# One core: a first head that prepares itself differently, and a last head whose weighted sum goes by halves

## What is computed

```python
# q, k, v: (2, 8, 768, 64), proj: (64, 6)
q_bits = (q @ proj > 0); k_bits = (k @ proj > 0)
mask = bucket(q_bits)[..., :, None] == bucket(k_bits)[..., None, :]
scores = where(mask, q @ k.T / 8, -1e9)
attn = softmax(scores); x = attn @ v            # -> (1536, 512)
logits = x @ w_gate                             # (1536, 8)
# by falling logit: a token goes to its expert while that has < 192 tokens
y[tok] = relu(x[tok] @ w1[e]) @ w2[e]           # w1: (8, 512, 1024), w2: (8, 1024, 512)
h = y @ w_in; out = (h * sigmoid(h)) @ w_out    # w_in: (512, 2048)
```

## Time and profile before

| what | value |
|---|---|
| three executions, median | 775.11 us (773.96 to 776.61) |
| the profiled execution | 777.72 us, span 775.9 us |
| mean granted TensorE clock | 0.990 |
| PE busy | 744.7 us (96%) |
| DVE busy | 481.1 us (62%) |
| ACT busy | 268.1 us (35%) |
| POOL busy | 156.4 us (20%) |

### The profile page before, as it was taken

How to read it: one execution, slowest core, us unless ns; L and a number is a source line. 1 busy time by engine, 2 the same in 40 slices (tenths; PEclk the granted TensorE clock), 3 DMA queues, 4 the chain that set the end, 5 groups by cost and what they waited for, 6 DMA issues and landing times.

```text
span 775.9 us, 19348 instructions
## 1 busy us (share of the span) xinstructions
PE 744.7 (96%) x7778; PEld 629.4 (81%) x7785; DVE 481.1 (62%) x1097; ACT 268.1 (35%) x551; POOL 156.4 (20%) x193
## 2 busy tenths in 40 slices
PE   8799999999998899999999999999999999999996
PEld 4577777777777569999999999978887888878885
DVE  4788888888889888797797740653233323242321
ACT  4768767767765012222222212221013101211111
POOL 5443545545643011010010000000002000010001
PEclk9899999999999899999999999999999999999999
DMA  7265565565533063463463477500001000010001
GB/s 151 46 121 119 123 139 118 122 139 126 114 106 86 22 236 112 137 219 136 137 206 149 136 247 277 183 0 1 1 1 54 0 0 0 0 54 0 0 0 54
DMA packets 58194, 75.07 MB, mean 97 GB/s; under 512 B 28736, under 2 KB 43072, under 8 KB 57120
## 3 DMA queue, kind: packets, MB, share of 16 engines
q1 hardware_dynamic: 54592, 67.12, 30.3%
q0 software_dynamic: 2208, 7.21, 2.9%
q10 hardware_dynamic: 1344, 0.04, 0.1%
HBM read 64.92 MB, written 6.29 MB: 92 GB/s over the span
## 4 chain that ended last, share of the span: by engine, by line
PE 86%; issue 4%; DVE 3%; DMA 2%; ACT 2%; POOL 1%; DVEq 0%; SPq 0%; ACTq 0%; POOLq 0%
PE quad_ps L1527 17%; PE quad_ps L1416 10%; PE quad_ps L1428 10%; PE quad_ps L1249 9%; PE score_ps L1510 8%; PE quad_ps L1510 8%; PE score_ps L1234 5%; PE score_ps L1235 4%; PE work_ps L1358 3%; PE work_ps L1220 2%; PE quad_ps L1258 2%; DMA area<-x_rows,ids_now 1%; DMA experts_w<-in_k 1%; PE pv_ps L1202 1%; DVE area L1030 1%
## 5 line engine op out<-in xcount | busy, mean ns | idle before, releaser
L1527 PE MATMUL quad_ps<-y_s,w_in_s 128*128 128x512 f32 x576 | 137.8, 390 | 2.7 <-DVE y_s L1152 2.0
L1527 PEld LDWEIGHTS quad_ps<-y_s,w_in_s 128*128 128x128 f32 x576 | 107.9, 188 | 26.2 <-DVE y_s L1152 2.8
L1170 DVE TENSOR_TENSOR gate<-quad_ps,sig 128x512 f32<-128x512 f32 x48 | 33.2, 692 | 145.9 <-ACT sig L656 145.9
L870 DVE TENSOR_SCALAR_CACHE_REDUCE att_area<-score_ps 128x768 f32<-128x768 f32 x96 | 91.9, 957 | 39.1 <-PE score_ps L1235 37.4
L524 ACT ACTIVATE att_area<-att_area 128x768 f32<-128x768 f32 x96 | 90.1, 939 | 46.0 <-DVE att_area L870 44.8
L656 ACT ACTIVATE sig<-quad_ps 128x512 f32<-128x512 f32 x48 | 28.7, 598 | 210.5 <-PE quad_ps L1527 210.5
L1416 PE MATMUL quad_ps<-area,experts_w 128*128 128x192 f32 x512 | 96.1, 334 | 1.5 <-ACT area L616 1.2
L1428 PE MATMUL quad_ps<-area,experts_w 128*128 128x192 f32 x512 | 87.2, 328 | 0.0
L1416 PEld LDWEIGHTS quad_ps<-area,experts_w 128*128 128x128 f32 x512 | 81.8, 190 | 2.1 <-ACT area L616 2.1
L1428 PEld LDWEIGHTS quad_ps<-area,experts_w 128*128 128x128 f32 x512 | 82.9, 190 | 0.0
L1234 PE MATMUL score_ps<-k_parts,q_parts 128*128 128x512 f32 x192 | 72.9, 380 | 10.3 <-DVE att_area L870 10.0
(11 more groups left out here) (204 smaller groups left out, 1104.6 us busy)
## 6 DMA issues: line engine op xcount, KB each, us to landing
experts_w<-in_moe_w SPq DMA_DIRECT2D x16, 2048.0 KB, 9.5
att_area<-in_v SPq DMA_DIRECT2D x64, 192.0 KB, 3.8
experts_w<-in_moe_w_in SPq DMA_DIRECT2D x8, 512.0 KB, 5.4
w_out_raw<-in_moe_w_out SPq DMA_DIRECT2D x4, 1024.0 KB, 8.3
experts_w<-in_k SPq DMA_DIRECT2D x16, 192.0 KB, 3.3
experts_w<-in_q SPq DMA_DIRECT2D x16, 192.0 KB, 3.6
k_bits<-k_parts SPq DMA_DIRECT2D x16, 192.0 KB, 4.6
x_rows<-att_area SPq DMA_DIRECT2D x8, 384.0 KB, 3.1
```

The lines of the kernel that those rows point to most:

```text
L870: nc.vector.tensor_scalar(probs[c % 3], score_ps[0][:, 0:S], 0.5 * BIG, None, ALU.min, ALU.min, accum_out=neg_max[:, c:c + 1]).then_inc(s_ ...
L1170: nc.vector.tensor_tensor(gate[:, :], layer_ps[f % 2][:, 0:GT], sig[:, :], ALU.mult).then_inc(s_mul, 1)
L1527: done = nc.tensor.matmul(layer_ps[f % 2][:, 0:GT], w_in_s[:, a, w_cols], y_s[:, c, b, :], start=(c == 0 and a + b == 0), stop=(c == DC - ...
```

## The change

Front: the high part of q of head 0 is written by ScalarE instead of GpSimd; the two transfers of the gate weights are started by SP, behind those of v; TensorE gets unread products in the slots of the first pair (`FIRST_UNREAD`, per head and slot). End of attention: the weighted sum of head 14 is shared out as 8, 8, 0, 8 blocks over slots 0 to 3 of the last head instead of 4, 4, 0, 12, 4; ScalarE copies it a slot earlier, and both copies of the best row come after that; the weighted sum of head 15 is made for tiles 0 to 2 and then for tiles 3 to 5 (96 columns a product instead of 192), the first half as soon as three tiles are transposed; its copy and `x_rows` go by halves too, and the copy stands ahead of ScalarE's six drains of head 14 (L588). GpSimd makes the last two splits of `w_in` one after the other, ahead of the logits of head 13. First ranking: unread products after rows 5 to 10 are 4, 4, 4, 3, 2, 0 instead of 4 each.

```diff
--- before.py
+++ after.py
@@ -412,6 +412,8 @@
             cross(0, k_drained(0))
             load_v(0, 0)
             load_v(1, 1)
+            for r0 in (0, D):
+                sp.dma_start(to_x[r0:r0 + D, :, D:DE], w_gate.rearrange("(h d) e -> d h e", d=D)).then_inc(s_wg, 16)
             cross(1, k_drained(1))
 
             def pair(g, write):
@@ -525,20 +527,21 @@
                                      bias=neg_max[:, c:c + 1],
                                      accum_out=row_sum[:, c:c + 1]).then_inc(s_exp, 1)
 
-            def turned(h):
+            def turned(h, ts=slice(0, T)):
 
                 act.wait_ge(s_pv, h + 1)
-                nc.scalar.activation(weighted_t.rearrange("p (t a j) -> p a t j", t=T, j=Q), sums_ps, ACT.Copy).then_inc(s_turned, 1)
+                dst = weighted_t.rearrange("p (t a j) -> p a t j", t=T, j=Q)
+                nc.scalar.activation(dst[:, :, ts, :], sums_ps[:, :, ts, :], ACT.Copy).then_inc(s_turned, 1)
 
             for i in range(4):
                 drain_work(PREP_KINDS[i], i % 2, i, 0)
+            act.wait_ge(s_work_free, 6)
+            nc.scalar.activation(q_bits[0][0:D, :], q_parts[0][0:D, :].bitcast(f32), ACT.Copy).then_inc(s_bit_step, 1)
             for t in range(2):
                 exp_tile(t, t)
                 for half in range(2):
                     drain_work("q" if t else "k", half, PREP + 2 * t + half, 1)
             act.wait_ge(s_halves, 5)
-            for r0 in (0, D):
-                act.dma_start(to_x[r0:r0 + D, :, D:DE], w_gate.rearrange("(h d) e -> d h e", d=D)).then_inc(s_wg, 16)
 
             def first_batch_row_out(c):
 
@@ -554,7 +557,7 @@
                     for t in range(T):
                         c = p * T + t
                         n = 2 * T * g + c
-                        if t == T - 1 and not (first and p == 0):
+                        if t == (T - 2 if last and p == 1 else T - 1) and not (first and p == 0):
                             if not first:
                                 act.wait_ge(s_x_full, 2 * g + p - 1)
                             turned(2 * g + p - 1)
@@ -565,8 +568,9 @@
                             w = w + 1
                         if len(ev[t]) < 2:
                             next_exp(n, c, last)
-                        if last and p == 1 and t >= T - 2:
-                            first_batch_row_out(t - (T - 2))
+                        if last and p == 1 and t == T - 2:
+                            first_batch_row_out(0)
+                            first_batch_row_out(1)
 
             def next_exp(n, c, last):
 
@@ -581,13 +585,14 @@
             none = assigned[:, 0, 0:1].unsqueeze(1).broadcast_to([P, NT, 2 * P - CAP])
             nc.scalar.activation(one_hot[:, :, CAP:2 * P], none, ACT.Copy).then_inc(s_cleared, 1)
             act.wait_ge(s_x_full, HEADS - 1)
+            for half in range(2):
+                turned(HEADS - 1, slice(half * (T // 2), (half + 1) * (T // 2)))
             act.wait_ge(s_xw, 16 * PAIRS)
             act.wait_ge(s_head_logits, HEADS - 1)
             for t in range(T):
                 col = t * DE
                 x_half = nc.scalar.activation(x_nat[:, t, 0:D], work_banks[0][:, col:col + D], ACT.Copy, scale=row_inv[:, t:t + 1])
             x_half.then_inc(s_x_free, 1)
-            turned(HEADS - 1)
 
             def second_batch_row_out():
 
@@ -733,8 +738,7 @@
 
             def finish_first_bits():
 
-                keep_high_of_q(0, 6)
-                pool.wait_ge(s_bit_step, 1)
+                hold(s_work_free, 6)
                 nc.gpsimd.tensor_scalar(k_bits[0][D:P, :], k_bits[0][D:P, :].bitcast(f32), -BIG, k_shift[D:P, :],
                                         ALU.mult, ALU.add).then_inc(s_bit_step, 1)
                 pool.wait_ge(s_bit_step, 2)
@@ -784,11 +788,10 @@
                     if not last:
                         split_rows(h + 2, p, g + 1)
                     if last and p == 1:
-                        split_beside(PAIRS - 2, h)
+                        for i in (PAIRS - 2, PAIRS - 1):
+                            split_beside(i, h)
                     if not first:
                         add_logits(h - 2)
-                    if last and p == 1:
-                        split_beside(PAIRS - 1, h)
                     if beside is not None and p == 0:
                         split_beside(beside, h)
 
@@ -1210,15 +1213,16 @@
                                             start=False, stop=True)
                 last.then_inc(s_work_full, 1)
 
-            def x_rows(h, bank, free=None):
+            def x_rows(h, bank, free=None, ts=range(T)):
 
                 rhs = to_x[:, h % H, :] if isinstance(h, int) else to_x[:, bass.ds(h % H, 1), :].rearrange("p a e -> p (a e)")
                 if free is not None:
                     pe.wait_ge(s_work_free, free)
-                pe.wait_ge(s_turned, h + 1)
-                for t in range(T):
+                pe.wait_ge(s_turned, h + 1 + (ts[0] > 0))
+                for t in ts:
                     last = nc.tensor.matmul(bank[:, t * DE:(t + 1) * DE], weighted_t[:, t * P:(t + 1) * P], rhs, start=True, stop=True)
-                last.then_inc(s_x_full, 1)
+                if ts[-1] == T - 1:
+                    last.then_inc(s_x_full, 1)
 
             def scores(c, h, n, crossed):
 
@@ -1236,20 +1240,20 @@
                                             start=False, stop=True)
                 done.then_inc(s_scores, 1)
 
-            def weighted(h, p, b0, n, loads):
+            def weighted(h, p, b0, n, loads, t0=0, t1=T):
 
                 if n and b0 == 0:
-                    pe.wait_ge(s_pt, T * h + T)
+                    pe.wait_ge(s_pt, T * h + t1)
                     pe.wait_ge(s_v[p], 64 * loads + 64)
                     pe.wait_ge(s_turned, h)
                 for b in range(b0, b0 + n):
                     for a in range(P // Q):
                         rows = slice(Q * a, Q * (a + 1))
                         side = slice(D * (b % 2), D * (b % 2 + 1))
-                        done = nc.tensor.matmul(quad_ps[side, 512 * a:512 * a + QT],
+                        done = nc.tensor.matmul(quad_ps[side, 512 * a + Q * t0:512 * a + Q * t1],
                                                 v_quarters[p][rows, b % 4, D * (b // 4):D * (b // 4 + 1)],
-                                                probs_t[p][rows, :, Q * b:Q * (b + 1)], start=(b < 2), stop=(b >= KB - 2))
-                if n and b0 + n == KB:
+                                                probs_t[p][rows, t0:t1, Q * b:Q * (b + 1)], start=(b < 2), stop=(b >= KB - 2))
+                if n and b0 + n == KB and t1 == T:
                     done.then_inc(s_pv, 1)
 
             def keep_busy(n, bank, cols=512):
@@ -1286,7 +1290,9 @@
                     if j in (3, T - 1):
                         done.then_inc(s_row_ps, 1)
 
+            FIRST_UNREAD = [[1, 1, 4, 4, 2, 2], [0, 0, 3, 0, 0, 0]]
             SHARE = [4, 4, 0, 12, 4, 0]
+            LAST_SHARE = [8, 8, 0, 8, 0, 0]
 
             def pair(g, first, last):
                 u = prep_base(g)
@@ -1304,19 +1310,27 @@
                             fill_work(kind, half, u - 1, h + ahead, (p + ahead) % 2, work_banks[half],
                                       x_free=h if kind == "k" and half == 0 and not first else None)
                             u = u + 1
+                        if first:
+                            if p == 1 and t == 2:
+                                pe.wait_ge(s_work_free, u - 1)
+                            keep_busy(FIRST_UNREAD[p][t], idle_bank if p == 0 else work_banks[0])
                         if t == 2 and not first:
                             x_rows(h - 2, work_banks[0], u - 1)
                         if last and p == 1 and t == T - 2:
                             row_of_first_batch(u)
                         if len(ev[t]) < 2:
-                            weighted_part(h, p, t, first, g)
+                            weighted_part(h, p, t, first, g, LAST_SHARE if last and p == 1 else SHARE)
+                        if last and p == 1 and t == T - 1:
+                            pe.wait_ge(s_row, 2)
+                            x_rows(HEADS - 2, work_banks[0])
+                            weighted(HEADS - 1, 1, 0, KB, PAIRS - 1, 0, T // 2)
                         if last and (p == 0 and t >= T - 2 or p == 1 and t < 2):
                             keep_busy(2, work_banks[1])
 
-            def weighted_part(h, p, t, first, g):
+            def weighted_part(h, p, t, first, g, share=SHARE):
 
                 if not (first and p == 0):
-                    weighted(h - 1, 1 - p, sum(SHARE[0:t]), SHARE[t], g if p else g - 1)
+                    weighted(h - 1, 1 - p, sum(share[0:t]), share[t], g if p else g - 1)
 
             pair(0, True, False)
             pe.wait_ge(s_wg, 32)
@@ -1324,10 +1338,9 @@
             with pe.Fori(1, PAIRS - 1, 1) as g:
                 pair(g, False, False)
```

(9 more changed lines are left out.)

## The result

The changed kernel takes 780.91 us (median of 5 runs, 779.9 to 782.94) against 775.11 (773.96 to 776.8, 5 runs) for the kernel before on the same chip: ratio 1.0071 [1.0054, 1.0088], 5.8 us slower. The profiled execution of after took 780.21 us, that of before 777.72, so the profiles hold only 2.5 us of difference; before's lies 2.6 above its median.

What follows compares the result with a forecast made beforehand. TensorE was seen busy nearly everywhere, with two 6.8 us stretches at 1.2 GHz. Front 2.2, copy and x_rows 0.3 and ranking 1.0 (half, for the median) make 3.5 us off 775.11: 771.6 us, range 770.0 to 774.6.

Steps and rivals of the forecast that it cites:

- Step 1: Front, high part of the first q on ScalarE: first scores start earlier, gain 0.25 us.
- Step 2: Front, gate weights issued from SP: ScalarE's drain of the k bits no longer waits for issues, gain 0.25 us.
- Step 3: Front, unread products in the first pair: they cost 0.2 us and gain 1.9 by removing the slow-clock stretch.
- rival (b): The low clock only moves, to the placing after the ranking: 773.5 us, or 775 if both places fall; chance 0.12.
- Step 4: Last head, shares 8, 8, 0, 8: scores slip 1.2 us, later slots give it back; net 0, bounds -0.3 and +0.7.
- Rival (d): The last head's slots hold back s_row by their 1.2 us: 772.8 us; chance 0.10.
- Step 5: GpSimd's last w_in splits together: last subtraction some 2 us earlier, not on the path; 0, up to 0.5 if logits late.
- Step 6: End of attention, head 15's weighted sum by halves: 4.1 us, as before; bounds 3.9 and 8.3.
- Rival (c): Weighted sum: a tile round keeps its length with halved columns, 8.3 us, kernel 775.8, or 777.1 at 25 ns; chance 0.10.
- rounds of over 0.12 us: Sign of a wrong forecast in head 15's weighted sum, where a round of eight was predicted at 0.085 us.
- Step 7: After head 15's sum, copy and x_rows by halves: gain 0.33 us, bounds 0 and 0.5.
- Step 8: First ranking, fewer unread products: `load` follows VectorE directly, gain 1.9 us, 0 without a slow clock, 1.0 for the median.

Runs made afterwards that it cites:

- e11_handed: `e1_front` without the unread products in the first pair, so only high part of q on ScalarE and gate weights on SP; 774.54 us, 0.9978 of before.
- e7_no_unread: `e2_whole` without the unread products in the first pair; 774.51 us, 0.9991 of before, twelve runs from 771.7 to 778.92.
- e1_front: The changed kernel with only its front part, end of attention and ranking as before; 774.45 us, 0.9987 of before.
- e6_twice: The changed kernel with head 15's weighted sum made twice over at full width (192 columns), no halves in it; 779.94 us, 1.0058 of before.
- e2_whole: The changed kernel with head 15's weighted sum in one go of 192 columns instead of halves; 773.04 us, 0.997 of before.
- e9_lean: `e2_whole` without unread products in the last head's first two slots; 772.33 us, 0.9948 of before, and again 771.94 us, 0.9945.
- e8_old_rank: `e2_whole` with the ranking's unread products as before, 4 after each of rows 5 to 10; 772.8 us, 0.996 of before.
- e4_halves: The kernel before with only head 15's weighted sum by halves of 96 columns; 778.73 us, 1.0041 of before.
- e5_filled: The changed kernel with 16 unread 512-column products spread through head 15's halves, one behind every 24 pairs; 782.9 us, 1.0098 of before.

## Why the prediction was wrong, step by step

- *Step 1* held. Scores start 2.96 us after the k bits' first drain instead of 3.23: 0.27 for a predicted 0.25.
- *Step 2* held: L520 follows its product without an issue. Its gain shows only without unread products, where the fourth and fifth minimum lie 2.36 us apart (`e11_handed`) instead of 2.55. In after it is 2.55 again: the unread products take the 0.19 back, as the 0.2 of step 3 allowed.
- *Step 3* held in the profile, 1.93 us for the whole front (predicted 2.2), of which the three tiles give 1.84 (1.9). It was mis-sized for the median: 1.1 us timed alone. The low clock of the one profiled execution isn't in all of them, and `e7_no_unread` kept its clock without the products, so it isn't shown that these are what keeps it. In `e1_front` a stretch fell on head 15's sum (the 5.85 us above). That is like rival (b), but neither at its place nor for its reason, since that kernel has the old products in the ranking.
- *Step 4* held: the slots slip by 1.30 (predicted 1.2) and give back 1.50. Rival (d) is out.
- *Step 5*: nothing of it is on the path, as said. GpSimd's last subtraction ends 4.8 us earlier (241.03), not 2, and VectorE's L883 takes 0.13 us at 242.09 instead of 2.09.
- *Step 6* is the step that failed: "4.1, as before", measured 9.20, above its own upper bound of 8.3. Its reasoning on the round was nearly right. Of the 45 rounds of eight inside the three runs 23 take 0.083 us, for a predicted 0.085; the others take 0.09 to 0.14, and the mean is 0.10. That makes 0.9 of the 5.05 us; the gaps make the rest (0.32 + 1.99 + 1.88 from start to start).
  What it left out is that the number of instructions doubles while the time for them doesn't, so that their supply becomes the bound. Rival (c) named the nearest time (775.8 to 777.1, with a chance of 0.10), still 3.8 us or more short, and by another mechanism, a fixed length of the round. That mechanism is refuted by the 0.083 us against 0.163 at full width (`e6_twice`). The sign I had set as wrong, "rounds of over 0.12 us", didn't occur in the mean. The 25 ns rule of the Trainium skill ("TensorE: Matmul & The Clock Gate", section "Wait — 56ns, not 53.3ns?") made it 9.6 us, close to the 9.20; the trace doesn't agree with it on these tiles, where pairs come 12.4 ns apart. The nearness is luck: the 9.20 comes from the supply's 27 ns a pair.
- *Step 7* held: sum's end to logits takes 2.31 us in `e2_whole` instead of 2.57, a gain of 0.26 (predicted 0.33). In after it is hidden by x_rows at 1.2 GHz: 2.84 us instead of 1.57.
- *Step 8* held in its mechanism: `load` follows right behind VectorE's last addition, L866. Its size is less sure. In `e2_whole` L1058 comes 13.97 us after the logits, 1.92 less (predicted 1.9), but that execution had no low clock there, and by the prediction itself the gain would then be 0. With one, at lengths like that of the earlier trace rows, this stretch of `e9_lean` takes 14.42 us from logits to `load`, 1.5 less than before:
```profile
255.80:263.00 7.20, 6.89 (x73) 3.62 (x75) 7.08 (x17) 0.00 (x0) 0.00 (x0) 0.53 0.01 2
```
  With a shorter one it is 0.8 (`e8_old_rank`). For the median I took 1.0, and it was nothing.

All steps but 6 give 2.5 us in the median, where the sum had 3.5. Step 6 cost 5.05 us itself. The remaining 2.8 of the 7.8 between `e2_whole` and the change I put down, for the most part, to the slow clock behind the sum: in the two profiled executions its end to `load` takes 18.4 against 16.3 us, 2.1 more. In `e4_halves` nothing of the kind is left over. Whether the gaps bring the low clock about is not shown. The profiled execution of `e5_filled`, without gaps, kept its clock behind the sum (16.2 us to `load`), which speaks for it; but that of `e4_halves`, with one gap, kept it up to 260 us too, and `e2_whole` has a fall behind its ranking without any.

Open: by what rule a packet of instructions is requested. At 96 columns the next packet starts 1.1 us, or 88 to 92 pairs, into a piece; at 192 columns 1.4 and 1.7 us, or 65 and 80 pairs (`e6_twice`). Neither a fixed place nor a fixed time fits both, and no experiment moved it. Nor was it tried to pad the code so that a border of a piece falls elsewhere.

## What to carry to other kernels

Before splitting an unrolled run of short products, count instructions, not only columns: what halves the work of an instruction doubles their number, and here TensorE got no more than 256 of them per 3.5 us in such a run (per 3.9 to 4.1 us in `e6_twice`, where each takes longer). A wait that ends with "issue" on an engine that has its data is the sign, and the instruction queue's packets in that stretch tell whether it is their supply. A clock fall seen in one profiled execution should be priced by how often it comes, by the spread of the timed runs, before its removal is counted in full.

## What the runs showed of the hardware

- In these runs instructions of TensorE come in packets of 16,384 bytes (256 instructions), each 0.9 to 1.2 us in transfer, and the run behind a gap starts 2.3 to 2.7 us after the packet started (after, `e4_halves`, `e6_twice`).
- On 32x64 tiles pairs of weight load and product of 96 columns come 12.4 ns apart in a run of 128, and 10 ns in half of its rounds of eight; with 192 columns they come 20 to 22 ns apart.
- A full-array product of 512 columns between tiled products costs 0.51 us, against 0.22 among its like: 0.32 in its own row of the chain, and the rest at the start of the tiled ones. Why is open.
- The clock of the same front was at 1.00 in the profiled execution of `e7_no_unread` and at 0.53 for 6.9 us in that of `e11_handed`.
